# u of four batches by seven block products, and o, k'v and mean squares in one visit

## The chip, the cores and the metric

The kernel runs on one core of one Trainium2 chip. The metric is the device time of one execution in microseconds, the median of several; before the change it is 788.39 us (three runs, 788.38 to 789.29). The profiled execution is another one: 788.02 us, with a span of 786.2 us in the trace. The engines have short names in the profile: PE is TensorE (PEld its weight loads), DVE is VectorE, ACT is ScalarE, POOL is GpSimd, SP is SyncE, which only issues DMAs.

## The reference

Batch 8, sequence 576, 8 heads of 64 (together 512). Three stages follow each other, all in float32:

```
kv  = einsum('bhsd,bhse->bhde', k, v);  out = einsum('bhsd,bhde->bhse', q, kv)
x   = out / sqrt(mean(out*out, -1) + 1e-6) * g_norm          # (b, s, 512)

h   = relu(x @ w_in)                                          # w_in 512 x 1024
u,v = h[..., :512], h[..., 512:];  v_n = (v - mean(v)) / sqrt(var(v) + 1e-6)
x   = (u * (einsum('ts,bsd->btd', w_spatial, v_n) + b_spatial)) @ w_out

h   = relu(x @ w_in2)                                         # w_in2 512 x 1024
out = (h * sigmoid(conv3(h))) @ w_out2                        # conv over the sequence, 3 taps
```

## The kernel before

**Split operands.** A float32 operand is kept as a high part (ScalarE rounds it) and a low part (VectorE subtracts), and a product has three passes: high x high, high x low, low x high. In every split, `_hi` is ScalarE's instruction and `_lo` VectorE's.

**Two phases.** Phase one makes the gated activations of all 8 batches, one `body(b)` each, from 40.35 to 405.90 us of the trace. It is followed by phase two (`body2`), whose x @ (w_out w_in2) is done in seven block products instead of eight (Strassen-Winograd: `PRODUCTS`, seven products of 6 steps, with sums of blocks on VectorE afterwards, `LAST_SUM`). w_out w_in2 is made in the prologue. The T operands of phase two (T1 to T4, differences of blocks of the gated activations) are made by VectorE at the end of each body (`t_a`, `t_b`, `t_c`) and stored to memory.

**A body, on TensorE** (L518). v of batch b in five tiles of rows, in the order 0, 1, 2, rest (64 rows), 3 (`V_TILES`); a tile is 12 steps of 128x512, the rest tile 8. Behind tile 0 stand the o blocks 0 and 1 of batch b+1, behind tile 2 the o blocks 2 and 3 (`o_product`, 8 small matmuls each); behind tile 3 the mean squares of batch b+1 (`square_sum`, 32 small matmuls) and k'v of batch b+2 (`kv_product`, 80 small matmuls; body 6 and 7 have none). Then u of batch b: four row blocks of 24 steps of 128x288 (`u_product`), 96 in all; and the gate products: four of 28 steps (`spatial_product`), 112. PSUM has 8 banks; each product waits until its banks were read.

**A body, on ScalarE** (L755) **and VectorE** (L1139). For each v tile: ScalarE does relu (`v_relu`), VectorE the statistics (`v_stats`: bn_stats, copy, bn_aggr, ve), ScalarE the root (`v_root`), VectorE four tiny operations and the scaling (`v_normalise`), ScalarE the high part (`v_hi`), VectorE the low part (`v_lo`). The rest tile has one more round: ScalarE copies a half, VectorE adds, ScalarE does relu; and it has two high copies. v's buffers are two, so a relu waits for the v_lo two tiles before. ScalarE copies the o blocks (`o_copy`) and squares them (`square`). VectorE makes the inverse root of batch b+1's mean squares (`inverse_root`), SP spreads it through memory (`spread_r`), VectorE scales x (`x_scale`); `x_hi` and `x_lo` split it. ScalarE does u's relu (`u_relu`), VectorE the gates (`gate`: gate product times u). k'v is copied half by ScalarE, half by VectorE (`kv_copy`).

**What sets the order.** Every engine's order is written out by hand; there is no planner. Engines wait for each other through counting semaphores (`s_vlo`, `s_g`, ...), and an instruction that waits holds everything behind it on its engine. SP's queue is in order too: q's load, the spread of r, k'v's load, the stores of the gated blocks. In bodies 1 and 2 w_out2 is loaded, split and stored to memory by the way (`wo2_load`, `wo2_split`, `wo2_low`, `wo2_store`), on ScalarE, its queue, and VectorE.

Of the kernel before, what the change touches and what calls it, by code (L numbers as in the profile page):

```python
# [59 lines left out]


# [10 lines left out]
GROUPS = FT // 2  # L72
PER_BATCH = NPROD * GROUPS

# [6 lines left out]
def build(nc, q_T, kv_main_dram, kv_rest_dram, consts, w_in, w_sp_T, b_sp, w_out_T, w_in2, w_out2, wo2_dram, op_dram, r_dram, out):  # L81
    with ExitStack() as ctx:
# [104 lines left out]
        selT = sb("head_spread", [P, CH * MT, D])  # L187
# [36 lines left out]
        s_T, s_To = map(sem, ("s_T", "s_To"))  # L224
        s_go = [sem("s_go0"), sem("s_go1"), sem("s_go2")]
# [7 lines left out]
        s_odr = sem("s_odr")  # L233

# [7 lines left out]
        def _(sp):  # L242
# [79 lines left out]
            sp.wait_ge(s_u, B * MT)  # L322
# [81 lines left out]
        def _(pe):  # L404
# [18 lines left out]
            def o_product(a, m):  # L423
                for half in (0, 1):
                    r = slice(half * D, (half + 1) * D)
                    for c in range(CH):
                        last = pe.matmul(PS[c * D:(c + 1) * D, O_BANK[m] + half, 0:HALF], kvd[r, m, c, :], QR[r, m, c, :],  # L427
                                         start=True, stop=True)
                last.then_inc(s_o, 1)
# [65 lines left out]
            def u_product(b, m, ahead):  # L495
                if m == 1:
                    pe.wait_ge(s_vr, b * NT + 4)
# [7 lines left out]
            def spatial_product(b, m):  # L505
                if m == 0:
                    pe.wait_ge(s_vlo, (b + 1) * NT)
                    pe.wait_ge(s_ur, b * MT + 1)
                if m == 1:
                    pe.wait_ge(s_ur, b * MT + 2)  # L510
                if m == 2:
                    pe.wait_ge(s_ur, b * MT + 4)
# [3 lines left out]
                wide(GATE_PAIR[m], steps).then_inc(s_sp, 1)  # L516

            def body(b, ahead, two_ahead):  # L518
                first = isinstance(b, int) and b == 0
# [10 lines left out]
                if two_ahead:  # L530
                    kv_product(b + 2)
                if first:
                    pe.wait_ge(s_winu, MT)
                for m in range(MT):
                    if m == 3 and two_ahead:
                        pe.wait_ge(s_kvd0, b + 3)
                        pe.wait_ge(s_kvd1, b + 3)
                    u_product(b, m, ahead)
# [3 lines left out]
                for m in range(MT):  # L542
                    spatial_product(b, m)
# [134 lines left out]
        def _(act):  # L678
            def kv_copy(a):
                act.wait_ge(s_kv, a + 1)  # L680
                act.wait_ge(s_o, a * MT)
                for half in (0, 1):
                    last = act.activation(kvd[half * D:(half + 1) * D, :, 0, :],
                                          PS[0:D, KV_BANK, 0:MT * D].rearrange("p (m e) -> p m e", m=MT), ACT.Copy)
                last.then_inc(s_kvd0, 1)

            def o_copy(a, m):
                act.wait_ge(s_o, a * MT + m + 1)
                act.wait_ge(s_xr, a)
                act.activation(whole(o_T[:, m, :]), PS[:, O_BANK[m]:O_BANK[m] + 2, 0:HALF], ACT.Copy).then_inc(s_oc, 1)  # L690
# [14 lines left out]
            def x_hi(a, m):  # L705
                act.wait_ge(s_xm, a * MT + m + 1)
                if m == 0:
                    act.wait_ge(s_u, a * MT)
# [4 lines left out]
            def v_relu(b, p):  # L713
                i, v = V_TILES[p], v_sb[p % 2]
# [16 lines left out]
            def v_root(b, p):  # L731
                n = P if V_TILES[p] < FULL else REST
# [3 lines left out]
            def v_hi(b, p):  # L736
                i, v = V_TILES[p], v_sb[p % 2]
# [6 lines left out]

            def u_relu(b, m):
                act.wait_ge(s_u, b * MT + m + 1)
# [8 lines left out]
            def body(b, ahead, two_ahead):  # L755
                first = isinstance(b, int) and b == 0
                for i in range(NT):
                    v_relu(b, i)
# [708 lines left out]
```

## Time and profile before

The page of the profile has these sums:

| | |
|---|---|
| median of the runs / profiled execution / its span | 788.39 / 788.02 / 786.2 us |
| busy: PE, DVE, ACT | 780.0 (99%), 583.1 (74%), 422.0 (54%) us |
| granted TensorE clock | full in all 40 slices |
| bodies 1 to 5, from first v step to next first v step | 46.79 or 46.80 us each |
| body 6; body 7 | 44.31; 40.28 us |
| VectorE adds 288 columns, one from PSUM (L1286) | 450 ns |
| VectorE subtracts 576 columns (L1186, L1087) | 755, 775 ns |
| VectorE copies half of k'v (L1042), two a batch | 427 ns each |
| VectorE subtracts 512 columns (L1130) | 685 ns |
| VectorE's idle time before x_scale of batch 0 (L1077), the longest | 2.5 us |

How to read it: the span is filled by TensorE; a busy share of 99% means that the other engines' idle time costs nothing, and that the sum of TensorE's instructions is the time. The durations in the lower half are means of one instruction; two instructions of one engine that don't depend on each other overlap a little, so that the distance from start to start is smaller.

### The profile page before, as it was taken

How to read it: one execution, taken by the hardware profiler on the slowest of the kernel's cores; microseconds unless marked ns; L12 is line 12 of the kernel's file. 1: busy time of each engine (PE TensorE's matmuls, PEld its weight loads, DVE VectorE, ACT ScalarE, POOL GpSimd, SP SyncE). 2: the span in 40 equal slices, each digit the busy share in tenths (PEclk: the TensorE clock that was granted, in tenths of full speed). 3: DMA queues.
4: the chain of work that ended last, by engine and by line, in shares of the span. 5: the costliest groups of instructions: out<-in, count | busy, mean ns of one | idle time of the engine just before them, and what ended most of it. 6: DMA issues, size and time to landing. Idle time of an engine off the chain costs nothing.

```text
span 786.2 us, 15138 instructions
## 1 busy us (share of the span) xinstructions
PE 780.0 (99%) x5654; PEld 702.3 (89%) x5654; DVE 583.1 (74%) x1262; ACT 422.0 (54%) x753; POOL 29.5 (4%) x40
## 2 busy tenths in 40 slices
PE   9999999999999999999999999999999999999997
PEld 7679899897988979899999898998989899898986
DVE  3765875866477484757899899497986979689791
ACT  4664452635335263432457757375774747567562
POOL 4342000000000000000000000000000000000000
PEclk9999999999999999999999999999999999999999
DMA  9872738575261642222092202231021212102102
GB/s 327 306 254 63 270 96 302 179 246 208 61 225 61 195 150 61 107 59 107 8 360 90 107 24 105 68 106 54 20 108 46 105 53 105 54 14 105 54 0 67
DMA packets 35005, 96.92 MB, mean 123 GB/s; under 512 B 2738, under 2 KB 9106, under 8 KB 30228
## 3 DMA queue, kind: packets, MB, share of 16 engines
q1 hardware_dynamic: 33476, 90.09, 33.7%
q10 hardware_dynamic: 1488, 6.30, 2.1%
q8 instruction: 23, 0.38, 0.2%
q14 instruction: 18, 0.15, 0.1%
HBM read 66.11 MB, written 30.28 MB: 123 GB/s over the span
## 4 chain that ended last, share of the span: by engine, by line
PE 96%; DMA 1%; DVE 1%; ACT 1%; SPq 1%; issue 0%; ACTq 0%; DVEq 0%
PE ps L458 28%; PE ps L643 25%; PE ps L635 21%; PE ps L484 11%; PE ps L427 2%; PE ps L411 2%; PE ps L491 2%; PE ps L562 1%; DMA work<-w_out_T_dram 1%; PE ps L437 1%; DVE h_and_sums L1286 0%; DVE t_then_s L1186 0%; PE ps L550 0%; SPq L279 0%; PE ps L450 0%
## 5 line engine op out<-in xcount | busy, mean ns | idle before, releaser
L643 PE MATMUL ps<-w_in_split,v_hg_split 128*128 128x512 f32 x832 | 194.9, 389 | 0.0
L643 PEld LDWEIGHTS ps<-w_in_split,v_hg_split 128*128 128x128 f32 x832 | 155.7, 188 | 32.3
L458 PE MATMUL ps<-w_sp_split,v_hg_split 128*128 128x288 f32 x896 | 120.1, 295 | 0.0
L458 PEld LDWEIGHTS ps<-w_sp_split,v_hg_split 128*128 128x128 f32 x896 | 119.3, 188 | 0.0
L458 PE MATMUL ps<-x_operand_split,w_in_split 128*128 128x288 f32 x768 | 103.8, 295 | 0.0
L458 PEld LDWEIGHTS ps<-x_operand_split,w_in_split 128*128 128x128 f32 x768 | 102.1, 188 | 0.7 <-issue 0.2
L484 PE MATMUL ps<-w_in_split,x_operand_split 128*128 128x512 f32 x384 | 92.0, 392 | 0.0
L484 PEld LDWEIGHTS ps<-w_in_split,x_operand_split 128*128 128x128 f32 x384 | 71.1, 188 | 17.3 <-issue 3.1
L1137 DVE TENSOR_TENSOR work<-ps,work 128x576 f32<-128x576 f32 x32 | 24.1, 756 | 68.8 <-PE ps L458 68.6
L1286 DVE TENSOR_TENSOR h_and_sums<-h_and_sums,ps 128x288 f32<-128x288 f32 x160 | 68.5, 450 | 7.7 <-PE ps L635 7.2
L1286 DVE TENSOR_TENSOR h_and_sums<-work,ps 128x288 f32<-128x288 f32 x64 | 28.2, 450 | 46.8 <-PE ps L635 46.3
L635 PE MATMUL ps<-x_operand_split,w_combined 128*128 128x288 f32 x384 | 61.5, 295 | 0.0
L724 ACT ACTIVATE work<-ps 128x512 f32<-128x512 f32 x32 | 19.1, 597 | 75.8 <-PE ps L484 71.7
L926 ACT ACTIVATE h_and_sums<-h_and_sums 128x576 f32<-128x576 f32 x64 | 43.4, 678 | 29.4 <-DVE h_and_sums L1286 28.9
L635 PE MATMUL ps<-operand_more_split,w_combined_more 128*128 128x288 f32 x384 | 56.5, 295 | 0.3 <-DVE h_and_sums L1286 0.3
L635 PEld LDWEIGHTS ps<-x_operand_split,w_combined 128*128 128x128 f32 x384 | 54.7, 188 | 0.0
L635 PEld LDWEIGHTS ps<-operand_more_split,w_combined_more 128*128 128x128 f32 x384 | 52.9, 188 | 0.6 <-DVE h_and_sums L1286 0.6
L1329 DVE SCALAR_TENSOR_TENSOR work<-h_and_sums,const_cols,work 128x576 f32<-128x576 f32 x64 | 52.1, 813 | 0.3
L1323 DVE SCALAR_TENSOR_TENSOR work<-h_and_sums,const_cols,work 128x576 f32<-128x576 f32 x64 | 52.0, 813 | 0.0
L932 ACT ACTIVATE work<-h_and_sums,const_cols 128x576 f32<-128x576 f32 x64 | 49.7, 776 | 3.0
L1334 DVE TENSOR_TENSOR work<-h_and_sums,work 128x576 f32<-128x576 f32 x64 | 48.2, 753 | 0.3 <-ACT work L942 0.3
L753 ACT ACTIVATE work<-ps 128x576 f32<-128x576 f32 x32 | 20.8, 650 | 49.3 <-PE ps L458 49.2
(124 smaller groups left out, 1068.4 us busy)
## 6 DMA issues: line engine op xcount, KB each, us to landing
kv_raw<-kv_main_dram SPq DMA_DIRECT2D x8, 2048.0 KB, 9.8
q_raw<-q_T_dram SPq DMA_DIRECT2D x8, 1152.0 KB, 5.1
operand_scratch<-t_then_s SPq DMA_DIRECT2D x8, 1152.0 KB, 4.7
operand_raw<-operand_scratch SPq DMA_DIRECT2D x8, 1152.0 KB, 5.7
sq_then_r<-r_scratch SPq DMA_DIRECT2D x14, 576.0 KB, 7.0
operand_scratch<-work SPq DMA_DIRECT2D x24, 288.0 KB, 2.7
operand_more_raw<-operand_scratch SPq DMA_DIRECT2D x8, 864.0 KB, 7.3
w_out_split_scratch<-v_hg_split ACTq DMA_DIRECT2D x2, 2048.0 KB, 8.6
```

Source lines behind the costliest of these rows:

```text
L458: last = pe.matmul(pair[bank][:, c, :], st, mo[:, c * HALF:(c + 1) * HALF], start=(n == 0), stop=(n == len(steps) - 1))
L484: last = pe.matmul(PS[:, V_BANK[i], 0:F1], XG[:, a, m, i * P:(i + 1) * P], WA[:, w, m, F1:2 * F1], start=(n == 0), stop=(n == len(steps) - 1))
L635: last = pe.matmul(PS[:, n % 8, 0:HALF], st, mo, start=(i == 0), stop=(i == len(steps) - 1))
L643: last = pe.matmul(PS[:, ROW_BANK[i], :], x, wout2[:, w, F_ORDER[e], :], start=(e == 0 and n == 0), stop=(e == FT - 1 and n == len(PASSES) ...
L753: act.activation(whole(u_sb[m]), pair[U_PAIR[m]], ACT.Relu).then_inc(s_ur, 1)
L926: act.activation(h_sb[f][:, 1:S + 1], h_sb[f][:, 1:S + 1], ACT.Relu).then_inc(s_hr, 1)
L932: act.activation(t_sb[e % 2], h_sb[f][:, 1:S + 1], ACT.Copy, scale=cols[:, FT + f:FT + f + 1]).then_inc(s_t0, 1)
L1137: dve.tensor_tensor(whole(u_sb[m]), pair[GATE_PAIR[m]], whole(u_sb[m]), ALU.mult).then_inc(s_g, 1)
L1286: dve.tensor_tensor(dst, x, PS[:, (g * NPROD + k) % 8, 0:HALF], ALU.add).then_inc(s_sum, 1)
L1323: dve.scalar_tensor_tensor(out=t, in0=h_sb[f][:, 0:S], scalar=cols[:, f:f + 1], in1=t, op0=ALU.mult, op1=ALU.add).then_inc(s_cv1, 1)
L1329: dve.scalar_tensor_tensor(out=t, in0=h_sb[f][:, 2:S + 2], scalar=cols[:, 2 * FT + f:2 * FT + f + 1], in1=t, op0=ALU.mult, op1=ALU.add).th ...
L1334: dve.tensor_tensor(p_sb[e % 2], h_sb[F_ORDER[e]][:, 1:S + 1], p_sb[e % 2], ALU.mult).then_inc(s_mul, 1)
```

## The change

Three things change, all in phase one.

1. **u in seven products (bodies 3 to 6; `FAST` = 3).** u = x @ w_u is cut into 2 x 2 blocks (256 x 256 weight blocks, 256 x 288 x blocks). The seven products have 6 steps of 128x288 for each of two groups of 128 rows: 84 steps instead of 96. The combined weights S1 to S4 are made once (sums in the prologue, split in body 1). The T blocks of x are made in every body before, by VectorE (`u_t_raw`, 4 operations; `u_t_lo`) and ScalarE (`u_t_hi`); T4 replaces a block of x itself, so it is split only when v is done. After the products, ScalarE copies the first one of a group (`u_first_copy`), and VectorE adds seven times a group (`u_sums`). The relu moves into the gate (`fast_gate`: max with 0, times the gate product), so `u_relu` goes.
2. **One visit (bodies 1 to 6; `v_visit`).** TensorE does v tiles 0 and 1, then all four o blocks, then k'v, then the mean squares, then the rest tile and tiles 2 and 3 (`VISIT_TILES`). ScalarE copies the four o blocks one after the other and squares two; VectorE squares the other two; ScalarE copies all of k'v. The inverse root moves ahead of the rest tile.
3. **TensorE's bodies 1 to 6 are written out** instead of a loop for bodies 1 to 5; ScalarE and VectorE loop over bodies 3 to 5.

Body 0 and body 7 keep their order. The core of the diff, with what the prediction speaks of:

```
+VISIT_TILES = [0, 1, FULL, 2, 3]
+VISIT_BANK = [6, 4, 2, 0]
+FAST_BANK = [6, 7, 1, 0, 2, 3, 4, 5]
+FAST_GATE = [2, 3, 0, 1]
+U_T_ORDER = [T2, T1, T3, T4]
...
+        u_operand[T4] = [XG[:, c, 0:2, HALF:S] for c in (HI, LO)]
...
@@ TensorE
+            def fast_product(b, g, k, ahead, two_ahead):
+                n = g * NPROD + k
+                if n == 2:
+                    pe.wait_ge(s_vr, b * NT + 2)
...
+                elif n == 5:
+                    pe.wait_ge(s_vr, (b + 1) * NT)
+                elif n == 6 and ahead:
+                    pe.wait_ge(s_ms, b + 2)
+                elif n == 7 and two_ahead:
+                    pe.wait_ge(s_kvd0, b + 3)
+                    pe.wait_ge(s_kvd1, b + 3)
+                elif n == 8:
+                    pe.wait_ge(s_ux1, b * U_GROUPS - FAST * U_GROUPS + 1)
+                elif n > 8:
+                    pe.wait_ge(s_usum, fast_u(b) + LAST_SUM[n - 8])
+                a, t = PRODUCTS[k]
+                if g == 0 and t in U_T_ORDER:
+                    pe.wait_ge(s_UTlo, fast_t(b) + U_T_ORDER.index(t) + 1)
+                steps = [(u_weight[a][w][:, j, g * P:(g + 1) * P], u_operand[t][x][:, j, :]) for j in (0, 1) for w, x in PASSES]
+                for i, (st, mo) in enumerate(steps):
+                    last = pe.matmul(PS[:, FAST_BANK[n % 8], 0:HALF], st, mo, start=(i == 0), stop=(i == len(steps) - 1))
+                last.then_inc(s_up, 1)
...
+            def v_visit(b, two_ahead):
+                v_product(b, 0, False)
+                v_product(b, 1, False)
+                o_ready(b + 1, 1)
+                o_product(b + 1, 0, VISIT_BANK)
+                o_product(b + 1, 1, VISIT_BANK)
+                pe.wait_ge(s_g, b * MT)
+                o_product(b + 1, 2, VISIT_BANK)
+                pe.wait_ge(s_vr, b * NT + 2)
+                o_product(b + 1, 3, VISIT_BANK)
+                pe.wait_ge(s_oc, (b + 1) * MT + 2)
+                if two_ahead:
+                    kv_product(b + 2)
+                square_ready(b + 1)
+                square_sum(b + 1)
+                pe.wait_ge(s_xr, b + 1)
+                pe.wait_ge(s_oc, (b + 2) * MT)
+                v_rest_product(b)
+                v_product(b, 2, False)
+                v_product(b, 3, False)
...
-            body(0, True, True)
-            with pe.Fori(1, B - 2) as b:
-                body(b, True, True)
-            body(B - 2, True, False)
-            body(B - 1, False, False)
+            body(0, True, True, False, False)
+            for b in range(1, B - 1):
+                body(b, True, b + 2 < B, b >= FAST, True)
+            body(B - 1, False, False, False, False)
@@ ScalarE
+            def v_visit(b, two_ahead, fast):
+                v_relu(b, 0, VISIT_TILES)
+                v_root(b, 0, VISIT_TILES)
+                v_relu(b, 1, VISIT_TILES)
+                for m in range(MT):
+                    o_copy(b + 1, m, VISIT_BANK)
+                square(b + 1, 0)
+                square(b + 1, 2)
+                v_hi(b, 0, VISIT_TILES)
+                v_root(b, 1, VISIT_TILES)
+                if two_ahead:
+                    kv_copy(b + 2, True)
+                v_hi(b, 1, VISIT_TILES)
+                root(b + 1)
+                if isinstance(b, int) and b in (1, 2):
+                    wo2_load(b - 1)
+                v_relu(b, 2, VISIT_TILES)
+                v_root(b, 2, VISIT_TILES)
+                v_relu(b, 3, VISIT_TILES)
+                v_hi(b, 2, VISIT_TILES)
+                v_root(b, 3, VISIT_TILES)
+                v_relu(b, 4, VISIT_TILES)
+                if fast:
+                    u_t_hi(b, T4)
+                v_hi(b, 3, VISIT_TILES)
+                v_root(b, 4, VISIT_TILES)
+            def fast_body(b, two_ahead, make_t):
+                v_visit(b, two_ahead, True)
+                u_first_copy(b, 0)
+                v_hi(b, NT - 1, VISIT_TILES)
+                u_first_copy(b, 1)
+                for m in range(MT):
+                    x_hi(b + 1, m, True)
+                if make_t:
+                    for t in U_T_ORDER[:3]:
+                        u_t_hi(b + 1, t)
@@ VectorE
+            def u_t_raw(a):
...
+                if isinstance(a, int) and a == FAST:
+                    dve.wait_ge(s_wo2_st, 2 * DMA)
+                u_t_block(raw[T1], x12, x11)
...
+            def u_add(b, g, dst, x, k, product):
+                dve.wait_ge(s_up, fast_u(b) + g * NPROD + product + 1)
+                dve.tensor_tensor(dst, x, PS[:, FAST_BANK[(g * NPROD + k) % 8], 0:HALF], ALU.add).then_inc(s_usum, 1)
+            def u_sums(b, g):
...
+                dve.wait_ge(s_ux1, b * U_GROUPS - FAST * U_GROUPS + g + 1)
+                if g:
+                    own(0)
+                else:
+                    for s in s_go:
+                        dve.wait_ge(s, DMA * b)
+                    dve.wait_ge(s_T, b * 4)
+                u_add(b, g, a_u2, a_x1, 1, 1)
+                u_add(b, g, top[:, 0:HALF], a_x1, 2, 2)
...
+            def v_visit(b, fast):
+                v_stats(b, 0, VISIT_TILES)
+                v_normalise(b, 0, VISIT_TILES)
+                v_stats(b, 1, VISIT_TILES)
+                square(b + 1, 1)
+                square(b + 1, 3)
+                if fast:
+                    u_t_lo(b, T3)
+                v_lo(b, 0, VISIT_TILES)
+                v_normalise(b, 1, VISIT_TILES)
+                mean_square(b + 1)
+                v_lo(b, 1, VISIT_TILES)
+                inverse_root(b + 1)
+                v_stats(b, 2, VISIT_TILES)
+                v_normalise(b, 2, VISIT_TILES)
+                v_stats(b, 3, VISIT_TILES)
+                v_lo(b, 2, VISIT_TILES)
+                v_normalise(b, 3, VISIT_TILES)
+                v_stats(b, 4, VISIT_TILES)
+                if fast:
+                    u_t_lo(b, T4)
+                v_lo(b, 3, VISIT_TILES)
+                v_normalise(b, 4, VISIT_TILES)
+            def fast_body(b, two_ahead, make_t):
+                v_visit(b, True)
+                u_sums(b, 0)
+                v_lo(b, NT - 1, VISIT_TILES)
+                u_sums(b, 1)
+                for m in range(MT):
+                    x_scale(b + 1, m)
+                fast_gate(b, 0)
+                for m in range(MT):
+                    x_lo(b + 1, m)
+                fast_gate(b, 1)
+                if make_t:
+                    u_t_raw(b + 1)
+                fast_gate(b, 2)
+                if make_t:
+                    u_t_lo(b + 1, T2)
+                    u_t_lo(b + 1, T1)
+                fast_gate(b, 3)
+                t_a(b)
+                t_b(b)
+                t_c(b)
...
             inverse_root(0)
+            u_combine_weights(0)
             dve.wait_ge(s_const_in, DMA)
             x_scale(0, 0)
```

In the plain bodies 1 and 2 VectorE keeps its order behind the v tiles, with `u_t_raw` of batch 3 between `x_lo` and gate 2 of body 2, and the low parts of T2 and T1 behind gate 2.

## Rows read from the trace of the kernel before

**Rows 1.** Windows of bodies 3 and 6: busy time (instructions) by engine, clock, DMA.
```profile
180.93:227.72 46.79, 46.79 (x409) 42.18 (x409) 30.09 (x76) 19.46 (x37) 0.00 (x0) 1.00 0.46 146
...
321.31:365.62 44.31, 44.31 (x329) 39.77 (x329) 29.07 (x74) 18.64 (x35) 0.00 (x0) 1.00 0.25 75
```
**Rows 2.** Chain that ended last, in order of time: start us, us, what.
```profile
183.67 1.13 PE ps L427 x16
184.80 5.66 PE ps L484 x24
...
199.95 27.77 PE ps L458 x208
...
365.62 8.18 PE ps L484 x36
...
378.33 27.57 PE ps L458 x208
...
450.83 22.39 PE ps L635 x168
```
**Rows 3.** Timeline of ScalarE in body 3: start us, us, line, operation [idle before].
```profile
183.71 0.60 ACT L724 ACTIVATE work<-ps 128x512 f32<-128x512 f32 x1 [9.12 <-PE ps L484]
184.38 0.65 ACT L690 ACTIVATE o_x<-ps 128x576 f32<-128x576 f32 x1
...
191.86 0.69 ACT L699 ACTIVATE sq_then_r<-o_x 128x576 f32<-128x576 f32 x1
192.45 0.62 ACT L740 ACTIVATE v_hg_split<-work 128x512 fp32r<-128x512 f32 x1
...
197.61 0.20 ACT L734 ACTIVATE vsd<-ve 64x1 f32<-64x1 f32 x1 [0.68 <-DVE ve L1108]
...
206.54 0.65 ACT L753 ACTIVATE work<-ps 128x576 f32<-128x576 f32 x1 [2.39 <-PE ps L458]
207.09 0.62 ACT L740 ACTIVATE v_hg_split<-work 128x512 fp32r<-128x512 f32 x1
```
**Rows 4.** Timeline of ScalarE in body 7, the rest tile's first high copy.
```profile
382.44 0.63 ACT L742 ACTIVATE v_hg_split<-work 64x512 fp32r<-64x512 f32 x1 [0.60 <-DVE work L1123]
```
**Rows 5.** Timeline of VectorE in body 3.
```profile
188.41 0.70 DVE L1103 BATCH_NORM_STATS2 bn_stats<-work 128x6 f32<-128x512 f32 x1 [0.65 <-ACT work L724]
...
189.49 0.68 DVE L1130 TENSOR_TENSOR v_hg_split<-work,v_hg_split 128x512 fp32r<-128x512 f32 x1
190.09 0.16 DVE L1114 RECIPROCAL vr<-vsd 128x1 f32<-128x1 f32 x1
...
190.92 0.55 DVE L1123 TENSOR_SCALAR work<-work,mean_var,vrs 128x512 f32<-128x512 f32 x1
191.38 0.69 DVE L1103 BATCH_NORM_STATS2 bn_stats<-work 128x6 f32<-128x512 f32 x1
...
195.06 0.68 DVE L1101 TENSOR_TENSOR work<-ps,work 64x512 f32<-64x512 f32 x1
196.44 0.69 DVE L1103 BATCH_NORM_STATS2 bn_stats<-work 64x6 f32<-64x512 f32 x1 [0.70 <-ACT work L729]
...
203.83 1.06 DVE L1062 RECIPROCAL r<-std 128x144 f32<-128x144 f32 x1
...
205.87 0.31 DVE L1070 TENSOR_TENSOR r<-r,std 128x144 f32<-128x144 f32 x1
```
**Rows 6.** Timeline of VectorE in body 7, behind the rest tile's low part.
```profile
384.34 0.16 DVE L1114 RECIPROCAL vr<-vsd 128x1 f32<-128x1 f32 x1
```
**Rows 7.** Timeline of TensorE in phase two: a late sum, and twelve steps elsewhere.
```profile
420.63 1.87 PE L635 MATMUL ps<-operand_more_split,w_combined_more 128*128 128x288 f32 x12 [0.34 <-DVE h_and_sums L1286]
...
426.33 1.76 PE L635 MATMUL ps<-operand_more_split,w_combined_more 128*128 128x288 f32 x12
```
**Rows 8.** DMA issues of the page: count, KB each, median us to landing.
```profile
w_out_split_scratch<-v_hg_split ACTq DMA_DIRECT2D x2, 2048.0 KB, 8.6
```

More of the change, by code:

```diff
@@ L515, in spatial_product, with v_turns @@
                 steps += [(vnA[:, d], wspA), (vnB[:, d], wspB)]
-                wide(GATE_PAIR[m], steps).then_inc(s_sp, 1)
-            def body(b, ahead, two_ahead):
-                first = isinstance(b, int) and b == 0
+                wide((FAST_GATE if fast else GATE_PAIR)[m], steps).then_inc(s_sp, 1)
+            def v_turns(b, ahead, two_ahead):
                 for i in V_TILES:
@@ new lines, in fast_body, with body @@
+            def fast_body(b, two_ahead, make_t):
[8 more added lines that the diff above has]
+                        u_t_hi(b + 1, t)
+            def body(b, ahead, two_ahead, make_t):
+                first = isinstance(b, int) and b == 0
+                visit = ahead and not first
+                if visit:
+                    v_visit(b, two_ahead, False)
+                else:
+                    for i in range(NT):
+                        v_relu(b, i)
+                        if ahead and i in (0, 2):
+                            o_copy(b + 1, i)
+                            square(b + 1, i)
+                        if i:
+                            v_hi(b, i - 1)
+                        if first and i >= 2:
+                            sp_hi(i - 2)
+                        if ahead and i == NT - 1:
+                            root(b + 1)
+                        v_root(b, i)
+                        if ahead and i in (0, 2):
+                            o_copy(b + 1, i + 1)
+                            square(b + 1, i + 1)
+                    if two_ahead:
+                        kv_copy(b + 2)
@@ L792, in body @@
                         x_hi(b + 1, m)
+                    if isinstance(b, int) and b == 1:
+                        for n in range(4):
+                            u_weight_hi(n)
+                    if make_t:
+                        for t in U_T_ORDER[:3]:
+                            u_t_hi(b + 1, t)
                 else:
@@ new lines, in body @@
+            def body(b, ahead, two_ahead, make_t):
+                visit = ahead and not (isinstance(b, int) and b == 0)
+                tiles = VISIT_TILES if visit else V_TILES
+                if visit:
+                    v_visit(b, False)
+                else:
+                    for i in range(NT):
+                        v_stats(b, i)
+                        if ahead and i == NT - 1:
+                            mean_square(b + 1)
+                        if i:
+                            v_lo(b, i - 1)
+                        v_normalise(b, i)
+                    if two_ahead:
+                        kv_copy(b + 2)
+                    if ahead:
+                        inverse_root(b + 1)
@@ L1168, in body @@
                         x_lo(b + 1, m)
+                    if isinstance(b, int) and b == 1:
+                        for n in range(4):
+                            u_weight_lo(n)
+                    if make_t:
+                        u_t_raw(b + 1)
                 else:
```

277 lines of the change are left out of this document (189 added, 88 removed).

## The prediction

> **What bounds the kernel now.** I read the windows first, one per body of phase one. In each, the matmul busy time equals the window: 46.79 us in a body with k'v, 44.31 us in body 6, which has none. VectorE is busy for 30.09 us and ScalarE for 19.46 us [rows 1]. TensorE waits for nobody there, so the end moves with TensorE's own work, and any wait that enters a body moves it too. The chain of waits then gives the price list. A 128x512 step of v costs 8.18 / 36 = 0.227 us. The 24 steps between two visits to the o blocks take 5.66 us, not 5.45: 0.21 us is paid on leaving the o blocks. 208 steps of u and gate take 27.57 us behind v (body 7) and 27.77 us behind k'v: 0.20 us on leaving k'v. One step is 0.1325 us. Seven products of six steps, four times over, take 22.39 us: 0.80 us a product [rows 2].
>
> **The change, part by part.**
>
> *Seven products for u (bodies 3 to 6).* 96 steps become 84: 12.72 us become 14 x 0.80 = 11.20 us, so -1.52 us a body if nothing waits.
>
> *One visit to o, k'v and mean squares (bodies 1 to 6).* ScalarE's first o copy starts 0.67 us behind its relu, so the first o block takes 0.67 us of the pair's 1.13 us and the second 0.46 us [rows 2, 3]: 0.21 us is paid on entry. One entry (0.21), one exit (0.21) and the exit from k'v into u (0.20) go: -0.62 us. The new steps from o into k'v and from k'v into the mean squares have no row; each costs between 0 and 0.21 us, and I take 0, since both stages already contain one entry. Bodies 1 and 2 fall to 46.17 us. Their first u product begins at 18.60 us, counted like all times below from the body's start (before: 46.79 - 27.77 = 19.02; two of the three savings stand ahead of it).
>
> *Work added to VectorE in a fast body:* 14 sums over 288 columns at 0.45, and 2 squares, 4 raw T blocks and 4 low parts over 576 columns at 0.76; the k'v copies (0.87 us) leave. That is 6.3 + 7.6 - 0.9 = 13.0 us on top of 30.1 (durations as in the table of the profile before): 43 of some 46 us. As a sum it fits. What decides is the order.
>
> *What is late next.* TensorE's product 6 (A22 x T4, counted from 0) waits for T4's low part, which VectorE makes behind the statistics of the last v tile. I add up the chain that leads there. It begins at the end of v's second tile, at 24 x 0.227 = 5.45 us, and alternates between ScalarE and VectorE:
> (a) ScalarE: relu starts +0.04, first o copy +0.67, four copies at 0.55 (a 576 column copy out of PSUM, start to next start), two squares at 0.59, then v_hi(0) starts: 4.09 us [rows 3].
> (b) v_hi 0.62 + 0.03, v_lo to the reciprocal 0.60, reciprocal to scaling 0.83, scaling 0.55 + 0.03, v_hi(1) 0.65, v_lo(1) 0.60: 3.91 us [rows 3, 5].
> (c) inverse_root: 2.04 us to its last step, 0.24 for that: 2.28 us [rows 5].
> (d) The rest tile: add to statistics 1.38, statistics to root 1.17 [rows 3, 5], root 0.24, reciprocal to scaling 0.83, scaling 0.58: 4.20 us.
> (e) From its two high copies over v_lo to the next reciprocal 1.90 [rows 4, 6], to scaling 0.83, to the next statistics 0.46, from these to the low part behind them 1.08, that part 0.76, 0.04 to TensorE: 5.07 us [rows 5].
> Sum 19.55; product 6 starts at 5.45 + 19.55 = 25.00 us. Left alone it would start at 18.60 + 6 x 0.80 = 23.40 us. So TensorE waits 1.6 us there, and 0.10 us more to refill: behind its one late sum in the second phase twelve steps took 1.87 us, elsewhere 1.76 [rows 7]. Behind its start stand eight products, 6.40 us, and the gate products, 112 x 0.1325 = 14.85 us. Body: 25.00 + 0.10 + 6.40 + 14.85 = 46.35 us against 46.79: **-0.44 us**, instead of the -2.14 that the two savings promise. The chain starts at v's second tile, so the 0.62 us saved behind it are swallowed too.
>
> *The sums behind it.* Product 11 needs sum 6. VectorE reaches the first sum at 26.7 us (T4's low part at 24.2, v_lo(3) 0.67 later, then 0.60, 0.83 and 0.46), and sum 6 ends near 29.1, while product 11 would begin at 25.10 + 4.00 = 29.10. It just fits; up to 0.2 us a body if the seven waits ahead of the first sum cost time. I take 0. v_lo(4) follows at once, well before the gate products at 31.5. The r spread starts some 10 us earlier in the body; SP's queue issues it, and q's load, earlier, and nobody waits for either. ScalarE issues w_out2's load 8 us later in bodies 1 and 2, ahead of a need at about 27 us.
>
> *Body 6.* Having no k'v, it was 2.48 us shorter than its neighbours. Its chain (a) to (e) now has the same length, since k'v is in none of the terms: TensorE, through with o at 7.5 us, waits 2.1 us for the squares, then at products 5 and 6. Body 6 is 46.35 us as well, against 44.31: **+2.04 us**. This one body gives back all that the others win.
>
> *Bodies 2 and 3.* Body 2 adds the raw T blocks (2.8 us) ahead of gate 2, for which v's first tile of body 3 waits. Behind gate 1 (39.5 us) and x's low parts (3.05) VectorE ends gate 2 at 46.1; the body ends at 46.17: 0.05 us at most. Gate 3, the T blocks of the second phase and the statistics of body 3's first tile come 1 us later, and the root of that tile stands ahead of the relu on which chain (a) rests: +0.54 us in body 3.
>
> *Prologue.* Three sums of 512 columns between inverse_root(0) and x_scale(0): 1.9 us in VectorE's 2.5 us of idle time there. Taken as 0; without that cover 1.9 us, of which x has 0.7 us to spare before v needs it.
>
> **Sum.** -0.62 (body 1), -0.57 (2), +0.10 (3), -0.44 (4), -0.44 (5), +2.04 (6): +0.1 us. The profiled execution took 788.02 us, a span of 786.2 and 1.8 around it; the median of the runs is 788.39, 0.37 above. Forecast **788.5 us**, no change.
>
> The row of v_lo shows 0.68 us, and its successor starts 0.60 us behind its start [rows 5]: VectorE's instructions overlap by 0.08. The Trainium skill, VectorE: DVE Perf Modes, section The DRAIN you can't avoid, says that the next operation doesn't start until the pipe is empty. By that rule five places of the chain would grow by 0.08, 0.4 us a body and 1.7 us in four, and the time would be 790.1. The row speaks against it for these instructions.
>
> **Rivals.**
> *The handovers are longer* (slower). The chain has some 22 handovers, 12 of them between engines, and I took 0.03 to 0.04 us each. The kernel before has few instructions that wait for more than two semaphores; here up to seven waits stand ahead of one, which speaks for it. Against it: the terms are start to start in the same kind of code. At 0.02 more a handover a fast body grows by 0.44, at 0.04 by 0.9: 790.2 to 792.0. It decides once the mean is 0.02 above mine, because TensorE has no slack behind product 6.
> *The chain is shorter* (faster), by an overlap that I missed. Each 0.1 us a body is 0.4. The end is where T4 isn't late at all: bodies 3 to 5 at 44.65 us, body 6 held by the squares alone at 44.3, 780.8 us in all. Against that end: 1.6 of 19.55 us would have to go, and nearly every term is a row. Half a microsecond less gives 786.5.
> *The w_out2 store is late* (slower, one place). In body 2 VectorE waits for it before the raw T blocks, with gates 2 and 3 queued behind and TensorE behind gate 2. Issued at about 32.0 us, needed at 42.5: 10.5 us. A landing took 8.6 us in the median [rows 8]; the k'v load of 2 MB runs earlier now and shares the queues with its start. Each us beyond 10.5 costs one: 789.5 to 791.
>
> **Chances.** Forecast 0.43, shorter chain 0.25, longer handovers 0.25, late store 0.07. A measurement tells 0.2%, 1.6 us, from no change. The forecast's own range is 786.9 to 790.1. Faster 0.25, within 0.43, slower 0.32. Range of 8 in 10: 785.4 to 792.0; the cases beyond it are the far ends of the two rivals on the chain.
>
> **What the changed profile would show.** Bodies 1 and 2 near 46.2 us; 4, 5 and 6 near 46.35; body 6 with TensorE idle for 2 us ahead of the mean squares. In fast bodies one wait of about 1.6 us for VectorE's low part ahead of the seventh product, which starts 25.0 us behind the body's start. Wrong if TensorE idles elsewhere, if the granted clock leaves 1.00 behind such a wait, or if the chain's start isn't the relu of v's second tile.

## The result and the profile after

The changed kernel takes **790.51 us** (median of 14 runs, 789.07 to 792.10), the kernel before 788.66 us beside it (14 runs, 788.21 to 789.67): ratio 1.0021, 95% interval 1.0013 to 1.0028. The forecast was 788.5 us in a range of 785.4 to 792.0. The change makes the kernel slower by about the 0.2% that I had called the bound of no change; the interval reaches over it on both sides. One execution of an experiment below (short_chain_b6_old_t4_early) was a slow one, 840.92 us at a granted clock of 0.85, and stands in no median.

Below stand the windows of bodies 1 to 6 in the profiled execution after (791.5 us, span 789.6), each from the first v step to the next first v step; the columns are those of [rows 1]. Body 5 is left out: 46.60 us.

```profile
88.10:134.34 46.24, 46.24 (x411) 42.45 (x410) 35.34 (x84) 22.65 (x45) 0.00 (x0) 1.00 0.67 227
134.34:180.79 46.45, 46.39 (x410) 42.38 (x409) 35.84 (x85) 22.50 (x44) 0.00 (x0) 1.00 0.63 216
180.79:229.24 48.45, 46.80 (x397) 42.52 (x398) 42.26 (x100) 19.14 (x39) 0.00 (x0) 0.96 0.44 142
229.24:275.81 46.57, 45.05 (x398) 40.95 (x397) 41.12 (x98) 19.37 (x39) 0.00 (x0) 1.00 0.45 147
322.41:368.92 46.51, 44.05 (x318) 39.60 (x317) 36.86 (x92) 15.97 (x32) 0.00 (x0) 0.96 0.24 72
```

In [rows 1] TensorE's busy time equalled the window; in bodies 4 and 6 it is now 1.5 and 2.5 us short of it. The list of TensorE's waits (us in total, times, longest) names what it waits for:

```profile
PE ps L575 <- DVE x_operand_split L1354: 4.9, 4, 1.5
PE ps L483 <- ACT sq_then_r L811: 2.2, 1, 2.2
```

L575 is a block product, L1354 the low part of a T block, L483 the mean squares. The chain of waits through body 4 (start us, us, what; many short pieces left out) shows how the time is now made. Rows of [rows 2] in which TensorE followed TensorE have become an alternation of ScalarE and VectorE:

```profile
229.40 5.48 PE ps L530 x24
...
237.73 1.28 ACT sq_then_r L811 x2
...
241.58 0.64 ACT v_hg_split L855
...
242.85 1.06 DVE r L1244
...
245.11 0.69 DVE work L1283
245.82 0.64 ACT work L844
246.49 0.70 DVE bn_stats L1285
...
249.27 0.63 ACT v_hg_split L857
249.90 0.53 ACT v_hg_split L858
...
252.47 0.70 DVE bn_stats L1285
...
253.56 0.77 DVE x_operand_split L1354
...
254.47 6.65 PE ps L575 x48
261.12 14.85 PE ps L504 x112
```

Product 6 starts at 254.47 - 229.40 = 25.07 us behind the body's start. (The chain puts the body's first step at 229.40, where the gate steps before it end; in the timeline, and so in the windows, that step begins at 229.24. The forecast's times count as the chain does.) Body 3 has the same wait and is 1.9 us longer than body 4. TensorE's timeline of body 3 shows product 6 and the one behind it:

```profile
206.41 3.05 PE L575 MATMUL ps<-x_operand_split,w_in_split 128*128 128x288 f32 x12 [1.53 <-DVE x_operand_split L1354]
```

Two windows, around that wait and behind the one for the squares in body 6, show the granted clock (third column from the end):

```profile
203.00:212.00 9.00, 7.40 (x43) 6.96 (x42) 8.62 (x27) 3.34 (x7) 0.00 (x0) 0.81 0.69 188
330.00:338.00 8.00, 5.83 (x49) 4.53 (x46) 6.83 (x16) 4.20 (x9) 0.00 (x0) 0.79 0.06 21
```

Twelve steps took 3.05 us instead of the 1.76 of [rows 7], and the granted clock of that stretch is 0.81: a part of it ran at 1.2 GHz instead of 2.4. Behind the same wait of 1.5 us in bodies 4 and 5 the clock stayed at 1.00.

### The profile page after: what moved, and what is told of

Its sections match the earlier page's. It is cut to its first block, busy times and chain, and to the rows that moved or that the text cites. A ratio compares the mean times of both kernels' runs of the same rounds, so it can differ in the third digit from the quotient of the medians.

```text
span 789.6 us, 15170 instructions
## 1 busy us (share of the span) xinstructions
PE 774.9 (98%) x5606; PEld 699.9 (89%) x5606; DVE 637.0 (81%) x1360; ACT 421.1 (53%) x763; POOL 30.2 (4%) x40
## 4 chain that ended last, share of the span: by engine, by line
PE 78%; DVE 13%; ACT 4%; issue 3%; DMA 1%; SPq 1%; DVEq 0%; ACTq 0%
PE ps L754 25%; PE ps L746 21%; PE ps L504 17%; PE ps L530 6%; PE ps L575 4%; PE ps L674 1%; DMA work<-w_out_T_dram 1%; PE ps L473 1%; PE ps L457 1%; DVE bn_stats L1285 1%; DVE work L1305 1%; DVE t_then_s L1501 1%; PE ps L537 1%; DVE work L1393 1%; DVE v_hg_split L1312 1%
## 5 line engine op out<-in xcount | busy, mean ns | idle before, releaser
L530 PE MATMUL ps<-w_in_split,x_operand_split 128*128 128x512 f32 x384 | 90.4, 390 | 0.1
L504 PE MATMUL ps<-x_operand_split,w_in_split 128*128 128x288 f32 x384 | 51.6, 295 | 0.0
L504 PEld LDWEIGHTS ps<-x_operand_split,w_in_split 128*128 128x128 f32 x384 | 51.2, 188 | 0.3
L1119 ACT ACTIVATE work<-work 128x576 f32<-128x576 f32 x64 | 43.6, 681 | 2.3 <-DVE work L1646 1.8
L1657 DVE TENSOR_TENSOR v_hg_split<-work,v_hg_split 128x512 fp32r<-128x512 f32 x64 | 44.6, 696 | 0.0
```

Of the source, the lines that this page charges most:

```text
L504: last = pe.matmul(pair[bank][:, c, :], st, mo[:, c * HALF:(c + 1) * HALF], start=(n == 0), stop=(n == len(steps) - 1))
L530: last = pe.matmul(PS[:, V_BANK[i], 0:F1], XG[:, a, m, i * P:(i + 1) * P], WA[:, w, m, F1:2 * F1], start=(n == 0), stop=(n == len(steps) - 1))
L1119: act.activation(p_sb[e % 2], t_sb[e % 2], ACT.Sigmoid).then_inc(s_sig, 1)
L1657: dve.tensor_tensor(hg[LO][:, e, :], p_sb[e % 2][:, 0:w], hg[HI][:, e, :].bitcast(F32), ALU.subtract).then_inc(s_hlo, 1)
```

## The experiments

The eleven were timed in three groups, each on one chip and beside the kernel before; between the groups the ratios are to be compared, not the medians. The start of body 0 differs from one execution to the next, whatever the kernel (40.17 to 41.56 us in the traces used here), so the traces are compared from the first v step of body 0 to the end. The table has that time ("steady"), the bodies of the profiled execution, and the times.

| kernel | median (n) | ratio to before, interval | lowest clock of a run | steady | bodies 3, 4, 5, 6 |
|---|---|---|---|---|---|
| before (trace of [rows 1]) | 788.66 (14) | 1 | | 745.9 | 46.80, 46.79, 46.79, 44.31 |
| after | 790.51 (14) | 1.0021 [1.0013, 1.0028] | 0.996 | 748.4 | 48.45, 46.57, 46.60, 46.51 |
| before_unrolled | 788.41 (11) | 1.0 [0.9991, 1.0009] | 0.999 | 746.2 | 46.79, 46.80, 46.79, 44.31 |
| fill_waits | 789.70 (11) | 1.0016 [1.0007, 1.0025] | 0.999 | 746.9 | 46.95, 46.56, 46.56, 46.55 |
| t4_early | 789.58 (11) | 1.0012 [1.0003, 1.0022] | 0.996 | 747.0 | 46.97, 46.56, 46.57, 46.51 |
| b6_old_order | 786.99 (11) | 0.9987 [0.9978, 0.9996] | 0.998 | 744.6 | 46.95, 46.55, 46.52, 44.32 |
| visit_only | 788.20 (11) | 1.0 [0.9991, 1.0009] | 0.997 | 744.7 | 46.24, 46.23, 46.23, 45.97 |
| visit_only_fill | 787.43 (11) | 0.998 [0.9971, 0.9989] | 0.999 | 744.9 | 46.23, 46.24, 46.23, 45.88 |
| visit_only_b6_old | 786.08 (5) | 0.9964 [0.9951, 0.9978] | 0.999 | 743.6 | 46.23, 46.24, 46.23, 44.31 |
| short_chain | 788.01 (11) | 0.999 [0.9982, 0.9999] | 0.997 | 745.7 | 46.37, 46.19, 46.17, 46.61 |
| short_chain_b6_old | 785.74 (5) | 0.9963 [0.9951, 0.9976] | 0.999 | 743.3 | 46.34, 46.19, 46.06, 44.29 |
| short_chain_b6_old_t4_early | 786.0 (6) | 0.9967 [0.9955, 0.9979] | 0.999 | 743.3 | 46.38, 46.19, 46.06, 44.29 |
| shorter_chain_b6_old | 784.63 (5) | 0.9945 [0.9931, 0.9958] | 0.999 | 742.3 | 46.30, 45.63, 45.55, 44.29 |

The first four experiments of the table ran beside a kernel before of 788.45 us; visit_only, short_chain, short_chain_b6_old and short_chain_b6_old_t4_early beside one of 788.42; visit_only_fill, visit_only_b6_old and shorter_chain_b6_old beside one of 789.14.

**before_unrolled**: the kernel before, TensorE's bodies written out.

```
-            with pe.Fori(1, B - 2) as b:
+            for b in range(1, B - 2):
                 body(b, True, True)
```

> The kernel before, with TensorE's bodies 1 to 5 written out instead of looped; nothing else. Theory: instruction fetch costs nothing, same time (within 0.05%), first product of the weights at 17.4 us. Rival: the 0.9 us by which the changed kernel's prologue was late in its trace comes from the longer TensorE program; then this one is 0.5 to 1 us slower, and its prologue is late too.

788.41 against 788.45: writing out costs nothing in the median. The profiled execution starts late all the same: its first product of the weights stands at 18.65 us, not at 17.4 as expected, and body 0 at 41.54. This alone would leave the rival open. The traces of visit_only and b6_old_order, which are written out too, start body 0 at 40.17 and 40.46 us, and the latter has the whole prologue of the changed kernel. So neither the written-out program nor the change brings the later start of the changed kernel's profiled execution (41.20 against 40.28).

**fill_waits**: the changed kernel with dummy steps ahead of the two waits.

```
+            def idle_fill(bank, steps):
+                for i in range(steps):
+                    pe.matmul(PS[:, bank, 0:HALF], u_weight[S3][HI][:, 0, 0:P], u_operand[T3][HI][:, 0, :], start=True, stop=True)
...
+                if n == 6:
+                    idle_fill(FAST_BANK[n], 10)
...
                 if two_ahead:
                     kv_product(b + 2)
+                else:
+                    idle_fill(SSQ_BANK, 14)
```

> TensorE gets extra 128x288 steps that nobody reads: ten ahead of its wait for T4's low part in bodies 3 to 6 (1.33 us of a wait of 1.5), 14 ahead of the wait for the squares in body 6 (1.9 of 2.2). Theory 1 (the granted clock fell in bodies 3 and 6 because TensorE stood idle there, and in body 3 that cost 1.5 us of the end): clock 1.000 in all runs, body 3 at 46.9 instead of 48.45, bodies 4 to 6 unchanged at 46.5 although 1.3 us of work is added; median lower by 0.5 to 1.5 us. Theory 2 (the clock fell for another reason): clocks between 0.996 and 1.000 as before, time unchanged. If the waits aren't set by the other engines' chain, each filled body grows by up to 1.3 us.

The windows of its bodies 3, 4 and 6:

```profile
180.53:227.48 46.95, 46.77 (x406) 42.35 (x407) 42.05 (x100) 19.15 (x39) 0.00 (x0) 1.00 0.46 146
227.48:274.04 46.56, 46.44 (x408) 42.27 (x407) 41.11 (x98) 19.37 (x39) 0.00 (x0) 1.00 0.45 147
320.60:367.15 46.55, 46.24 (x343) 41.72 (x341) 36.84 (x92) 15.97 (x32) 0.00 (x0) 1.00 0.23 72
```

TensorE is busy nearly throughout, and bodies 4 and 6 are as long as they were with 1.5 and 2.5 us of idle time: their length is made elsewhere. Body 3 loses 1.5 us and is only 0.4 us longer than body 4. All eleven runs have a clock of 0.999 or 1.000, while of the changed kernel's fourteen runs three do (789.15 to 790.22) and eleven lie at 0.996 to 0.998 (median 790.87). The gain in the median is small: in ratios 1.0021 to 1.0016, 0.4 us, with intervals that overlap, where 0.5 to 1.5 us were expected.

**t4_early**: T4 is split some 2 us earlier on both engines.

```
@@ ScalarE
                 v_root(b, 3, VISIT_TILES)
+                if fast:
+                    act.wait_ge(s_v, (b + 1) * NT)
+                    u_t_hi(b, T4)
                 v_relu(b, 4, VISIT_TILES)
@@ VectorE
                 v_lo(b, 2, VISIT_TILES)
+                if fast:
+                    u_t_lo(b, T4)
                 v_normalise(b, 3, VISIT_TILES)
```

(The two later calls go.)

> T4 is split as soon as v's last product is done: ScalarE's high part ahead of the last relu, VectorE's low part behind v_lo(2), 2 us earlier than now. The amount of work on VectorE is the same. Theory (VectorE's order as a whole sets the end of u; T4 is only the first wait to show it): product 6 starts near 23.4 us of the body without a wait, and the wait moves to product 11, which needs sum 6 at 29.1 us: bodies 4 to 6 stay within 0.2 us of 46.55, median unchanged. Rival (T4's low part alone is late): bodies 3 to 6 lose the 1.5 us wait, 45.1 us each, median lower by some 5 us.

The wait moved, the body didn't shrink. It moved to another place than expected, to products 8 and 9 and not to product 11. TensorE's timeline in body 4: product 6 follows product 5 at once, and products 8 and 9 wait instead, for the first copy of product 0 (ScalarE) and for the first sum (VectorE).

```profile
251.80 1.76 PE L575 MATMUL ps<-x_operand_split,w_in_split 128*128 128x288 f32 x12
253.96 1.06 PE L575 MATMUL ps<-v_hg_split,operand_more_split 128*128 128x288 f32 x6 [0.41 <-ACT work L864]
255.69 1.06 PE L575 MATMUL ps<-x_operand_split,w_in_split 128*128 128x288 f32 x6 [0.66 <-DVE work L1359]
```

So T4's place in the order isn't the limit. That the whole of VectorE's and ScalarE's work between v's second tile and the first sums is, remains to be shown by short_chain and shorter_chain_b6_old.

**b6_old_order**: body 6 in the order and with the plain u of before, bodies 1 to 5 as changed.

```
-                body(b, True, b + 2 < B, b >= FAST, True)
+                body(b, True, b + 2 < B, FAST <= b < B - 2, b < B - 2)
@@ ScalarE, VectorE (dve alike)
-            with act.Fori(FAST, B - 2) as b:
+            with act.Fori(FAST, B - 3) as b:
                 fast_body(b, True, True)
-            fast_body(B - 2, False, False)
+            fast_body(B - 3, True, False)
+            body(B - 2, True, False, False)
```

> Body 6 goes back to the order of the kernel before (o behind v tiles 0 and 2, mean squares behind v, u in 96 steps); bodies 1 to 5 stay as changed. Theory (the chain through ScalarE and VectorE sets a fast body's length whether k'v is there or not, so body 6 alone gave 2.2 us away): body 6 falls from 46.51 to 44.3 us, the others stay, the median falls by 2.2 us to about 788.3. Rival (the loss sits in every fast body, or in the prologue, and body 6 lost only its clock): body 6 stays above 45.5 and the median falls by less than 1 us.

Body 6 returns to 44.32 us: -2.19, as expected. The median fell by more (in ratios 0.34%, 2.7 us). With the wait for the squares most of the falls of the clock went too (two of 11 runs below 0.999, before eleven of 14), which fits. This kernel is already faster than the one before, by 0.13%.

**visit_only**: u in the plain form everywhere, the new order kept. (`body(b, True, b + 2 < B, False, True)`, no T blocks, no combined weights.)

> u is made everywhere in the plain form of bodies 1 and 2 (no block products, no T blocks, no combined weights); the new order of the o blocks, k'v and squares behind v's second tile stays in bodies 1 to 6. Theory (the order alone is worth what body 1 shows, 46.79 - 46.23 = 0.56 us a body, and the block form's 24 steps fewer are eaten by the chain through ScalarE and VectorE): bodies 1 to 5 last 46.2 each, 5 x -0.56 = -2.8 against before; in body 6 the squares are waited for 2.17 us where k'v is missing, 46.23 - 2.55 + 2.17 = 45.9 against 44.31, +1.6. Sum -1.2: about 787.2 us, and bodies 3 to 5 are shorter by 0.3 than with the block form (46.55). Rival (the block form does earn its steps and the order costs): bodies 3 to 5 come out above 46.55, near the 46.8 of before or over it, and the sum is at or above 788.4.

Windows of bodies 4 and 6:

```profile
225.78:272.01 46.23, 46.23 (x411) 42.43 (x409) 30.64 (x76) 18.72 (x37) 0.00 (x0) 1.00 0.46 148
318.24:364.21 45.97, 43.80 (x331) 40.05 (x329) 30.56 (x76) 17.08 (x33) 0.00 (x0) 1.00 0.24 72
```

Both bodies came out as worked out. With 12 steps more, body 4 is **0.34 us shorter** than with the block products (46.57), and VectorE does 10.5 us less. The median was a miss, 788.20 instead of 787.2: four of its runs (clock 0.999 or 1.000) lie at 786.76 to 787.21, the seven others (0.997 or 0.998) at 788.15 to 790.00. Its only long wait in the bodies is this one:

```profile
328.14 1.19 PE L483 MATMUL ps<-sq_then_r,head_select 128*32 128x144 f32 x32 [2.17 <-ACT sq_then_r L811]
```

**visit_only_fill**: 14 dummy steps ahead of that wait.

```
                 if two_ahead:
                     kv_product(b + 2)
+                else:
+                    idle_fill(SSQ_BANK, 14)
```

> visit_only, and in body 6, where k'v is missing, TensorE does 14 dummy steps (their results are overwritten unread) ahead of its wait for the squares, which was 2.17 us. The bodies are otherwise those of visit_only, whose eleven runs lay between 786.76 and 790.00 with a mean granted clock of 0.997 to 1.000. Theory (the spread and the 1.2 us by which visit_only's median lay above what its bodies add up to are a granted clock that falls behind that one wait in some executions): body 6 stays at 45.97 within 0.1, every run shows a clock of 0.999 or 1.000, the median is 787.1 and none lies above 788. Rival (the fall has nothing to do with that wait): the runs spread as before, to 790, with clocks of 0.997, median 788.2.

TensorE's timeline in body 6, where the dummy steps (L553) now fill the time up to the squares:

```profile
326.56 2.12 PE L553 MATMUL ps<-x_operand_split,w_in_split 128*128 128x288 f32 x14
328.71 1.19 PE L483 MATMUL ps<-sq_then_r,head_select 128*32 128x144 f32 x32
```

The body is no shorter to speak of (45.88), yet all eleven runs have a clock of 0.999 or 1.000 and lie between 787.03 and 788.09, on a chip where the kernel before took 0.7 us longer than beside visit_only. In ratios the fill is worth 1.0 to 0.998, 1.6 us, with intervals that just don't meet (0.9991 and 0.9989). The median is 0.3 us above the expected 787.1, and one run lies above 788. So that single wait of 2.17 us brought the fall of the clock, and dummy work ahead of it kept the clock up.

**visit_only_b6_old**: the same, and `b < B - 2` for the last argument.

> visit_only with body 6 in the order of before: no block products anywhere, the new order in bodies 1 to 5 alone. Theory: 5 x -0.56 = -2.8 against before and body 6 back at 44.3, no wait of TensorE above 0.3 us in the batches' bodies: clock 0.999 or 1.000 in all runs, 785.6 us. So the block products with the shortened chain (785.74 measured in short_chain_b6_old) and none at all come out equal within 0.3 us. Rival (the block products earn something that this hides): this one is slower than 786.2.

786.08, ratio 0.9964, steady time 743.6: the best of the plain form. The median is 0.5 us above the expected 785.6, on a chip where the kernel before took 0.7 us more than in the group before. The block products with the shortened chain stand at 743.3 and 0.9963: equal, as expected.

**short_chain**: no work added or left out, three operations moved in bodies 3 to 6.

```
@@ ScalarE, bodies 3 to 6: behind the four o copies
+                v_root(b, 1, VISIT_TILES)
+                v_hi(b, 0, VISIT_TILES)
                 square(b + 1, 0)
                 square(b + 1, 2)
-                v_hi(b, 0, VISIT_TILES)
-                v_root(b, 1, VISIT_TILES)
@@ VectorE, bodies 3 to 6
                 square(b + 1, 3)
-                u_t_lo(b, T3)
                 v_lo(b, 0, VISIT_TILES)
...
-                v_stats(b, 2, VISIT_TILES)
+                v_stats(b, 2, VISIT_TILES, lambda: u_t_lo(b, T3))    # between the rest tile's add and its bn_stats
```

> The changed kernel with the chain of bodies 3 to 6 shortened: ScalarE takes the root of v's second tile and the high part of its first ahead of the squares, VectorE takes T3's low part while it would wait for the rest tile's statistics. No work is added or left out. Theory (the end of bodies 3 to 6 is set by that chain, not by TensorE's 45.0 us of steps and not by where T4 is split): the chain loses about 0.8 us, T4's blocks start at 24.3 instead of 25.07 behind the body's start, the wait of 1.53 us falls to 0.7, bodies 4 and 5 last 45.75 instead of 46.57; 4 x -0.8 = -3.2 where body 6 gains too, about 787.0 us, and the granted clock falls less often. Body 6 could gain less, since its wait for the squares (2.17 us) stands ahead of all that and grows by the 0.7 us of ScalarE's work that is now ahead of them. Rival (the time stands somewhere else, as it did when T4 alone was split 2 us earlier and the bodies stayed at 46.56): bodies stay at 46.5 and the sum at 790.

Right in kind, half in size: bodies 4 and 5 lose 0.38 and 0.43 us, not 0.8 (body 3 0.58, against 46.95 at full clock). The wait ahead of product 6 is 1.0 us instead of the expected 0.7. Two expectations failed: the median is 788.01, not 787.0, and the clock did not fall less often (nine of 11 runs at 0.997 or 0.998). Body 6 shows why. Its wait for the squares grows to 2.78 us, and in this execution the clock falls behind it:

```profile
330.89 3.43 PE L537 MATMUL ps<-w_in_split,rest_split 128*128 128x512 f32 x8
330.00:338.00 8.00, 8.00 (x49) 6.26 (x42) 5.98 (x16) 2.62 (x6) 0.00 (x0) 0.79 0.02 4
```

The eight steps took 3.43 us; in fill_waits, at full clock, they took 2.11. Here nothing hides that, for product 6 of body 6 no longer waits: the 46.61 us contain the longer wait and about 1.5 us of the clock. The two runs at full clock took 786.37 and 786.41 us, the nine others 787.69 to 788.75.

**short_chain_b6_old** and **short_chain_b6_old_t4_early**: both edits together, and all three.

> short_chain, and body 6 in the order of before with plain u. Theory: 786.99 (body 6 in the old order alone) less 3 x 0.8 in bodies 3 to 5: 784.6 us; body 6 lasts 44.3. Rival: bodies 3 to 5 stay at 46.5, 787.0.

> short_chain_b6_old, and T4 split ahead of v's fifth tile on ScalarE and behind the low part of the third on VectorE. Theory: T4 and v's last tiles end on one chain, so taking T4 forward only moves the wait behind product 6, as it did with the long chain (0.41 and 0.66 us there): bodies 3 to 5 last the same 45.75 as in short_chain_b6_old within 0.1, 784.6 us. Rival (T4's own place is what is left of the wait): the bodies fall to TensorE's own 45.1 to 45.3 and the sum to 783.0.

785.74 instead of 784.6: again about half of what was expected. The equality of the two (bodies within 0.04 us of each other) is as expected: T4's place is worth nothing with the shorter chain either.

**shorter_chain_b6_old**: the trace of short_chain_b6_old showed the missing half. VectorE had scaled v's second tile at 238.09 us, and ScalarE made its high part only at 238.71, behind four copies of k'v. Now, in bodies 3 to 5, two of the four stand behind the root of the mean squares.

```
-                    kv_copy(b + 2, True)
+                    kv_copy(b + 2, True, 0)
                 v_hi(b, 1, VISIT_TILES)
                 root(b + 1)
+                    kv_copy(b + 2, True, 1)
```

> short_chain_b6_old, and in bodies 3 to 5 ScalarE copies one half of k'v ahead of the high part of v's second tile and the other half behind the root of the mean squares, instead of all four copies ahead (they held that high part back by 0.6 us: VectorE's result was there at 238.09, the part began at 238.71). Theory (the chain through ScalarE and VectorE still sets the end of these bodies: 0.98 us of wait at T4's blocks are left): product 6 comes 0.58 us earlier, the wait falls to 0.4, bodies 3 to 5 from 46.34, 46.19 and 46.06 to 45.8, 45.6 and 45.5, the sum 785.74 - 1.7 = 784.0 us. Rival (another chain of equal length stands behind, as with T4 alone): bodies stay within 0.1 of what they were, 785.7.

The windows of its bodies 3 and 4:

```profile
180.87:227.17 46.30, 45.13 (x396) 40.96 (x397) 42.08 (x100) 19.18 (x39) 0.00 (x0) 1.00 0.45 149
227.17:272.80 45.63, 45.01 (x398) 40.90 (x397) 41.13 (x98) 19.52 (x39) 0.00 (x0) 1.00 0.46 150
```

And TensorE's timeline at product 6 of body 4:

```profile
251.44 1.83 PE L575 MATMUL ps<-x_operand_split,w_in_split 128*128 128x288 f32 x12 [0.41 <-DVE x_operand_split L1364]
```

Bodies 4 and 5 and the wait of 0.41 us came out as expected to 0.05 us; body 3 did not (46.30, expected 45.8; its wait is 0.86 us). VectorE enters body 3 late: its first statistics there start 4.8 us behind the body's start, in body 4 3.9 us. 784.63 us (expected 784.0), ratio 0.9945 [0.9931, 0.9958]: the fastest of all, and the first in which the block products earn something over the plain form. Beside visit_only_b6_old, on the same chip, it is 1.45 us faster; the five runs of either don't overlap (784.53 to 785.26, 785.66 to 786.56), and the steady time is 742.3 against 743.6.

## Why the forecast came out as it did

**What bounds the kernel, and where the 1.52 and 0.62 us go: right, and shown.** The forecast said that the end of bodies 3 to 6 moves from TensorE to a chain between ScalarE and VectorE, and put product 6 at 25.00 us; it started at 25.07. The parts agree as well, so that this isn't two errors that cancel: (a) to (e) were 4.09, 3.91, 2.28, 4.20 and 5.07 us, and took 4.00, 3.97, 2.26, 4.16 and 5.20 in body 4. The chain's end at T4 isn't the only one of that length (t4_early), and the 0.6 us that shorter_chain_b6_old takes out ahead of both ends is won nearly in full (0.56 and 0.51 us) in bodies 4 and 5. Filling the waits leaves the bodies as they are.

**The number: inside the range partly by luck.** 790.51 us lies above the forecast's own range (786.9 to 790.1), where I had given 0.32 to a slower kernel. It stands where the rival of longer handovers would have put it (790.2 to 792.0), but that mechanism gave 0.07 us. The room was left for one cause and filled by two others: about 1 us by which the bodies were summed too low, and the clock, which had no term.

**Bodies one by one**, forecast and measured against before: body 1 -0.62, -0.55; body 2 -0.57, -0.34; body 3 +0.10, +0.15 (with the clock at 1.00, as in b6_old_order); body 4 -0.44, -0.22; body 5 -0.44, -0.19; body 6 +2.04, +2.20. Sum +0.1, +1.05. Three terms were too small:
- *Behind product 6* I had 0.10 + 6.40 + 14.85 = 21.35 us; the chain has 6.65 + 14.85 = 21.50. With the 0.07 of the chain that is 0.2 us in bodies 4 and 5, and 0.16 in body 6. In body 3 it hardly shows, since VectorE's late start cost about 0.4 us over body 4 and not 0.54.
- *Body 2.* I had 0.05 us at most for the raw T blocks ahead of gate 2. In the trace gate 2 (L1393) runs from 179.89 to 180.64, and v's first step of body 3, which waits for it, follows at 180.79, some 0.2 us later than the gate steps alone would let it. visit_only, which has no T blocks, has 46.23 there.
- *Leaving the small tiles.* I took 0 for the two new passages, from the o blocks to k'v and on to the mean squares. Body 1, where only the visit changed, missed by 0.07 us: that is what both cost together at most. The Trainium skill, TensorEngine Tiling (Array Packing), section Key Properties, says that changing the tiling mode drains TensorE. The trace agrees for the way out of small tiles (0.2 us each, [rows 2]) and shows next to nothing between one small form and another.

**The clock: the step that was missing.** "Wrong if ... the granted clock leaves 1.00 behind such a wait" stood among the signs, but no term or rival had it. Without it the bodies alone give +1.05 us, and the runs at full clock (fill_waits) lie 1.25 us above before. The changed kernel lies 1.85 above. I put what remains, 0.6 to 0.8 us in the median (0.4 by the ratios), down to the clock, which is plausible and not clear of the noise in this pair. In the profiled execution the cost is plain: the clock fell twice, at a cost of 1.5 us in body 3 and of nothing in body 6, where the chain through the other engines had the slack (wait ahead of product 6 of 0.29 us there). In visit_only, where there is no such slack, the fill is worth 1.6 us.

**The rivals.** Longer handovers: no, 0.07 us in 22 of them. A shorter chain by overlap: no. A late w_out2 store: no. VectorE goes from x's last low part (L1272, at 176.76 for 0.42 us) to the first raw T block (L1337, at 177.09) without a gap, so it didn't wait for the store, and gate 2 was late by VectorE's own work. VectorE's overlap held: v_lo at 242.24 (0.69 us long), the reciprocal at 242.85, 0.61 us later as in [rows 5], so the 1.7 us that the rule of the Trainium skill (VectorE: DVE Perf Modes, section The DRAIN you can't avoid) would have given did not come. The same section says that a next operation that isn't held starts earlier, which I had left out; the rows agree with that.

## What to carry to other kernels

When TensorE fills the span and a change takes steps from it by giving work to other engines, write down the chain that leads from the last operand to the first product that needs it, start to start: it told the body's length to 0.2 us, and told that steps saved on TensorE behind the chain's start are worth nothing until the chain is shorter. Look for the iteration in which the neighbour work is missing (body 6 had no k'v): an order that is good where there is cover can cost more in that one iteration than it wins in all others. And give the waits a price beyond their length: in visit_only a dummy load ahead of a wait of 2 us cost nothing and won 1.6 us.

## What the runs showed of the hardware

- The granted clock fell behind waits of 1.5 and 2.2 us, in some executions and not in others of the same program: at 0.81 over the 9 us around product 6 of body 3, at 0.79 over 8 us in body 6 (there in the traces of t4_early and short_chain too), at 1.00 around the same waits in bodies 4 and 5. With the waits filled, 22 of 22 runs had 0.999 or 1.000. With the wait for the squares left in (2.2 to 2.8 us), 33 of 47 had 0.998 or less: 7 of 11 of visit_only, 6 of 11 of t4_early, 9 of 11 of short_chain, 11 of 14 of the changed kernel. With waits of 1.5 us alone (b6_old_order) it was two of 11 (788.60 and 789.13 us, against a median of 786.99), and with none above 1.0 us in the bodies none of 21 (the three kernels with a shortened chain and body 6 in the old order, and visit_only_b6_old). Why one execution falls and the next doesn't stays open, as does how often the clock fell in the slowest runs of visit_only: its traced execution has no fall.
- The start of body 0 moves by up to 1.4 us between executions (40.17 to 41.56 us in thirteen traces), and the kernel before comes near both ends: 40.28, and 41.54 written out.
